# A float32 attention + two-layer MoE kernel by seven-product matrix multiplication: reordering the first four steps of the second layer

## The reference

```python
# layer 1: x = (silu(xn @ w_gate) * (xn @ w_val)) @ w_out      512 -> 1536 -> 512
# layer 2, on 2304 tokens x 512:
h = x @ w_in                                                  # 512 -> 2048
g = np.where(h >= 1, h, np.where(h <= -1, 0.0, (h + 1) ** 2 / 4.0))
out = g @ w_out                                               # 2048 -> 512
```

## Time and profile before

| | |
|---|---|
| median of 3 runs | 873.04 us (872.49 to 873.92) |
| profiled execution, its own time | 873.55 us |
| span of its instructions | 871.8 us |
| mean granted TensorE clock | 0.996 |
| PE busy | 853.6 us, 98% of the span |
| DVE / ACT busy | 659.2 us (76%) / 490.2 us (56%) |
| steps 0 to 4 of the second layer | 491.93 to 560.02 us of the span |

### The profile page before, as it was taken

One profiled execution on the slowest core, in us unless ns is written; L12 is line 12 of the kernel. 1 busy time (PEld: TensorE's weight loads), 2 busy tenths in 40 slices (PEclk: granted clock), 3 DMA queues, 4 the chain that ended last, 5 costly groups with the idle time before them and its releaser, 6 DMA issues.

```text
span 871.8 us, 17848 instructions
## 1 busy us (share of the span) xinstructions
PE 853.6 (98%) x7332; PEld 831.7 (95%) x7332; DVE 659.2 (76%) x883; ACT 490.2 (56%) x736; POOL 162.7 (19%) x107
## 2 busy tenths in 40 slices
PE   8999999999999999999999998999999999999998
PEld 5888999999999999999999997899999889999998
DVE  4698966477954976987867986766667988988884
ACT  4566654445654665644434677777778944433331
POOL 1235263345764563000000000000000000000000
PEclk9999999999999999999999999999999999999999
DMA  9993232333336335355141013242436664444442
GB/s 251 253 266 88 77 103 90 92 101 104 103 103 205 110 103 199 110 163 163 31 134 49 2 56 102 111 157 109 158 141 220 199 203 145 122 123 140 126 122 72
DMA packets 109008, 113.46 MB, mean 130 GB/s; under 512 B 6784, under 2 KB 85696, under 8 KB 108928
## 3 DMA queue, kind: packets, MB, share of 16 engines
q1 hardware_dynamic: 108928, 112.33, 41.2%
HBM read 74.55 MB, written 37.75 MB: 129 GB/s over the span
## 4 chain that ended last, share of the span: by engine, by line
PE 87%; DVE 4%; ACT 3%; DMA 2%; issue 2%; SPq 1%; DVEq 0%; ACTq 0%
PE pair L794 17%; PE pair L796 16%; PE pair L795 16%; PE pair L988 5%; PE pair L990 5%; PE pair L989 5%; PE pair L884 5%; PE pair L886 5%; PE pair L885 5%; PE pair L738 2%; PE pair L749 2%; PE pair L686 2%; PE pair L960 1%; PE pair L959 1%; PE pair L712 1%
## 5 line engine op out<-in xcount | busy, mean ns | idle before, releaser
L794 PE MATMUL pair<-xc,wc 128*128 128x288 f32 x672 | 199.5, 297 | 0.2
L795 PE MATMUL pair<-xc,wc 128*128 128x288 f32 x672 | 198.2, 295 | 0.0
L796 PE MATMUL pair<-xc,wc 128*128 128x288 f32 x672 | 197.6, 294 | 0.0
L1130 ACT ACTIVATE cp<-pair 128x576 f32<-128x576 f32 x160 | 103.5, 647 | 158.8 <-PE pair L796 151.4
L2026 POOL TENSOR_TENSOR wc<-wt,wc 128x512 fp32r<-128x512 f32 x78 | 123.2, 1603 | 117.3 <-ACT wc L1057 85.9
L794 PE MATMUL pair<-xc,wr 128*128 128x288 f32 x448 | 134.1, 299 | 8.4 <-ACT cp L1130 8.4
L795 PE MATMUL pair<-xc,wr 128*128 128x288 f32 x448 | 133.6, 298 | 0.0
L796 PE MATMUL pair<-xc,wr 128*128 128x288 f32 x448 | 133.2, 297 | 0.0
L794 PEld LDWEIGHTS pair<-xc,wc 128*128 128x128 f32 x672 | 125.9, 187 | 1.1 <-issue 0.9
L796 PEld LDWEIGHTS pair<-xc,wc 128*128 128x128 f32 x672 | 126.6, 188 | 0.0
L795 PEld LDWEIGHTS pair<-xc,wc 128*128 128x128 f32 x672 | 126.2, 188 | 0.0
(11 more groups left out here) (154 smaller groups left out, 1689.3 us busy)
## 6 DMA issues: line engine op xcount, KB each, us to landing
b_scratch<-cb SPq DMA_DIRECT2D x32, 576.0 KB, 2.9
a_scratch<-cb SPq DMA_DIRECT2D x24, 576.0 KB, 2.9
y<-a_scratch SPq DMA_DIRECT2D x16, 864.0 KB, 5.9
wt<-wB SPq DMA_DIRECT2D x72, 128.0 KB, 2.9
bt<-b_scratch SPq DMA_DIRECT2D x28, 256.0 KB, 2.8
bt<-b_scratch SPq DMA_DIRECT2D x56, 128.0 KB, 3.0
a_k<-kT SPq DMA_DIRECT2D x16, 288.0 KB, 5.7
a_q<-qT SPq DMA_DIRECT2D x16, 288.0 KB, 5.0
```

The lines of the kernel that those rows point to most:

```text
L794: pe.matmul(o, wh, xh, start=FIRST[i] and j == 0, stop=False, skip_group_check=True)
L795: pe.matmul(o, wh, xl, start=False, stop=False, skip_group_check=True)
L796: mm = pe.matmul(o, wl, xh, start=False, stop=j == 1, skip_group_check=True)
L1130: act.activation(copied(g, n)[:, :, :], pair[(X, Q, X, X)[n]][:, :, 0:HALF], ACT.Copy).then_inc(s_c, 1)
```

## The change

In steps 1 to 3 the order of ACT's and DVE's instructions is another; that of step 0 and of the steps from 4 on comes out as before. On ACT, copies 2 and 3 come ahead of the parabolas and high parts that used to stand before them: in step 1 the high parts T2, B22 and parabola 2 now follow copy 2, parabola 3 stays behind copy 3; in step 2 the four high parts and parabola 2 follow copy 2 or copy 3; in step 3 the high parts T3, T4 of tile NT+3 are made between copies 1 and 2, and parabola 1 and 2 stand between copies 2 and 3 together with the first two weight parts. DVE's order follows that of ACT. The sums of unit 13 are made in two pieces, S1 and S3 at the end of step 2, S2 and S4 in step 3.

SP issues the load of unit 13 at the same place of its queue, but waits for other things: before, for all parts of tile NT+3 (the last tile), now for the low parts of tile NT+2. What used to be behind SP's wait is waited for in two places: DVE before the sum S1, ACT before the high part A11. So that the early load writes over nothing that is still read, the last four places of the ring are used in another order (`RING_END`): the raw values of A11 and A12 go to places 9 and 10, and S1 and S2 (which DVE writes later) to 7 and 8. The places of two parts of the last product's weights (`wa21_at`) move by one accordingly. No instruction is added or taken away but semaphore waits.

```diff
--- before.py
+++ after.py
@@ -39,6 +39,7 @@
 GALL = GB + GC
 UALL = 2 * UB + UC
 RING = 11
+RING_END = (9, 7, 10, 8)
 KH = FB // 2
 NBLK = NTOK // P
 
@@ -109,7 +110,8 @@
 
 def slot_of(un, i):
 
-    return (7 * (un - 2 * UB) + i) % RING
+    n = (7 * (un - 2 * UB) + i) % RING
+    return n if n < 7 else RING_END[n - 7]
 
 
 def last_quarter(T):
@@ -193,7 +195,7 @@
 
 
         wq_at = (z_xc, z_xc + XC + 512, z_xc2, z_copy2 + 2 * 15360 + 512)
-        wa21_at = (z_w + 8 * 4096, z_w + 9 * 4096, z_raw + 512, z_cl)
+        wa21_at = (z_w + 9 * 4096, z_w + 10 * 4096, z_raw + 512, z_cl)
         wqt = [place(f"wqt{r}", [7, 2, 2, WIDE], wq_at[r]) for r in range(NGRP)]
         wa21t = [place(f"wa21t{r}", [2, 2, WIDE], wa21_at[r]) for r in range(NGRP)]
         apart = [(wa21_at[r] - wq_at[r]) // 1024 for r in range(NGRP)]
@@ -591,15 +593,13 @@
                 n = g - GB
                 if n % NT == 2 and n < GC - 2:
                     un = unit_of(g) + 1
+                    sp.wait_ge(s_wl, 7 * un)
                     if n == 2:
 
-                        sp.wait_ge(s_xh, 7 * 2 * NT)
-                        sp.wait_ge(s_xlp, 3 * 2 * NT)
-                        sp.wait_ge(s_T, 4 * 2 * NT)
+                        sp.wait_ge(s_xlp, 3 * (2 * NT - 1))
                         sp.wait_ge(s_xld, 4 * (2 * NT - 1))
                     else:
                         sp.wait_ge(s_p, 7 * (g - 2))
-                    sp.wait_ge(s_wl, 7 * un)
                     load_unit(un)
                 if n == GC - 2:
                     load_b(0)
@@ -1309,11 +1309,9 @@
                 copy(g, 0)
                 if n == 0:
                     tile_hi(NT + 1, T1)
-                if n == 2:
-                    tile_hi(NT + 3, B11)
                 if n:
                     parabola(g - 1, 0)
-                if n > 2 and n != 4:
+                if n > 4:
                     parabola(g - 1, 1)
                 copy(g, 1)
 
@@ -1322,46 +1320,58 @@
                         tile_hi(NT + 1, i)
                 if n in (1, 2):
                     parabola(g - 1, 1)
+                if n == 2:
+                    tile_hi(NT + 3, B11)
+                if n == 3:
+                    tile_hi(NT + 3, T3)
+                    tile_hi(NT + 3, T4)
+                if n == 4:
+
+                    parabola(g - 1, 1)
+                elif n > 4:
+                    parabola(g - 1, 2)
+                copy(g, 2)
+                if n == 0:
+                    tile_hi(NT + 2, B11)
                 if n == 1:
                     tile_hi(NT + 2, T2)
                     tile_hi(NT + 2, B22)
                 if n == 2:
                     tile_hi(NT + 3, T1)
                     tile_hi(NT + 3, B21)
-                if n == 4:
-
+                if n == 3:
                     parabola(g - 1, 1)
-                elif n:
-                    parabola(g - 1, 2)
-                if n == 2:
-                    tile_hi(NT + 3, T2)
-                    tile_hi(NT + 3, B22)
-                copy(g, 2)
-                if n == 0:
-                    tile_hi(NT + 2, B11)
-                if n == 1:
-                    tile_hi(NT + 2, T3)
-                    tile_hi(NT + 2, T4)
-                if n == 3:
+                    act.wait_ge(s_xlp, 3 * 2 * NT)
+                    act.wait_ge(s_T, 4 * 2 * NT)
                     unit_hi(un + 1, A11)
                     unit_hi(un + 1, S1)
+                if n in (1, 2, 3):
+                    parabola(g - 1, 2)
                 if n == 4:
                     parabola(g - 1, 2)
                 if n == GC - 3:
                     plain_w_hi(0, (0,))
                 if n == GC - 1:
                     plain_w_hi(1, (0,))
-                if n:
+                if n > 3:
                     parabola(g - 1, 3)
                 copy(g, 3)
                 if n == 0:
                     tile_hi(NT + 2, T1)
                     tile_hi(NT + 2, B21)
+                if n == 1:
+                    parabola(g - 1, 3)
+                    tile_hi(NT + 2, T3)
+                    tile_hi(NT + 2, T4)
                 if n == 2:
-                    tile_hi(NT + 3, T3)
-                    tile_hi(NT + 3, T4)
+                    tile_hi(NT + 3, T2)
+                    tile_hi(NT + 3, B22)
+                    parabola(g - 1, 3)
                 if n == 3:
-                    for i in (A12, S2, S4, S3, A22):
+                    unit_hi(un + 1, A12)
+                    unit_hi(un + 1, S2)
+                    parabola(g - 1, 3)
+                    for i in (S4, S3, A22):
                         unit_hi(un + 1, i)
                 if n in (6, 10):
                     for i in (A11, S1, A12, S2):
@@ -1493,6 +1503,10 @@
             def unit_sum(un, s):
                 if s == S1:
                     dve.wait_ge(d_w[un % 2], 128 * (un // 2 + 1))
+                    if un == 2 * UB + 1:
+                        dve.wait_ge(s_xh, 7 * (2 * NT - 1) + B22 + 1)
+                        dve.wait_ge(s_xlp, 3 * 2 * NT)
+                        dve.wait_ge(s_T, 4 * 2 * NT)
                     dve.tensor_tensor(w_raw(un, S1), w_a21(un), w_raw(un, A22), ALU.add).then_inc(s_S, 1)
                 if s == S3:
                     if un >= 2 * UB:
@@ -1889,27 +1903,25 @@
             for g in range(GB, GALL):
                 un, n = unit_of(g), g - GB
                 if n == 2:
-                    tile_sums(NT + 3)
-                    token_lo(NT + 3, B11)
-                    token_lo(NT + 3, T1)
-                if n == 1 or n > 2:
+                    tile_sum(NT + 3, T1)
+                    tile_sum(NT + 3, T2)
+                if n:
                     joined(g - 1, 0)
-                if n == 3:
-                    unit_sums(un + 1)
                 c11(g)
                 if n == 0:
                     for i in range(B21, T4 + 1):
                         token_lo(NT + 1, i)
+                if n == 3:
+                    unit_sum(un + 1, S2)
+                    unit_sum(un + 1, S4)
+                else:
+                    if n:
+                        joined(g - 1, 1)
+                    if n > 3:
+                        joined(g - 1, 2)
                 if n == 2:
-                    joined(g - 1, 0)
-                    token_lo(NT + 3, B21)
-                if n:
-                    joined(g - 1, 1)
-                if n in (1, 2):
-                    token_lo(NT + 1 + n, T2)
-                    token_lo(NT + 1 + n, B22)
-                if n:
-                    joined(g - 1, 2)
+                    tile_sum(NT + 3, T3)
+                    tile_sum(NT + 3, T4)
                 if n in (GC - 3, GC - 1):
                     wq_sum((n - (GC - 3)) // 2, S1)
                     wq_sum((n - (GC - 3)) // 2, S3)
@@ -1917,27 +1929,53 @@
                 if n == 0:
                     tile_sums(NT + 2)
                 if n == 1:
-                    token_lo(NT + 2, T3)
-                    token_lo(NT + 2, T4)
+                    token_lo(NT + 2, T2)
+                    token_lo(NT + 2, B22)
+                if n == 2:
+                    token_lo(NT + 3, B11)
+                    token_lo(NT + 3, T1)
+                    token_lo(NT + 3, B21)
+                if n in (1, 2):
+                    joined(g - 1, 2)
+                if n == 3:
+                    unit_lo(un + 1, A11)
+                    unit_lo(un + 1, S1)
+                    joined(g - 1, 1)
                 if n in (6, 10):
                     unit_sums(un + 1)
-                if n in (3, 7, 11):
-                    for i in {3: (A11, S1)}.get(n, (A12, S2)):
+                if n in (7, 11):
+                    for i in (A12, S2):
                         unit_lo(un + 1, i)
-                if n:
+                if n > 3:
                     joined(g - 1, 3)
                 c22_c21(g)
                 if n == 0:
                     for i in (B11, T1, B21):
                         token_lo(NT + 2, i)
+                if n == 1:
+                    joined(g - 1, 3)
+                    token_lo(NT + 2, T3)
+                    token_lo(NT + 2, T4)
                 if n == 2:
+                    token_lo(NT + 3, T2)
+                    token_lo(NT + 3, B22)
+                    joined(g - 1, 3)
+                    unit_sum(un + 1, S1)
+                    unit_sum(un + 1, S3)
                     token_lo(NT + 3, T3)
                     token_lo(NT + 3, T4)
+                if n == 3:
+                    unit_lo(un + 1, A12)
+                    unit_lo(un + 1, S2)
+                    joined(g - 1, 2)
+                    joined(g - 1, 3)
+                    for i in (S4, S3, A22):
+                        unit_lo(un + 1, i)
                 if n in (6, 10):
                     unit_lo(un + 1, A11)
                     unit_lo(un + 1, S1)
-                if n in (3, 7, 11):
-                    for i in {3: (A12, S2, S4, S3, A22)}.get(n, (S4, S3, A22)):
+                if n in (7, 11):
```

(1 more changed line is left out.)

## The result

The changed kernel takes 861.59 us in the median (860.49 to 864.14, 4 runs) against 872.95 of the kernel before in the same measurement: ratio 0.9873, 95% interval 0.9849 to 0.9896. Forecast were 862.0 us and a range of 860.8 to 864.6. Two later measurements of the same kernel gave 861.73 (ratio 0.985, 0.9819 to 0.9881) and 861.87 (0.9866, 0.9841 to 0.9891).

What follows compares the result with a forecast made beforehand. PE, busy 98%, bounds the kernel; its waits, restarts and half clock in steps 0 to 4 lose 12.09 us. With 1.04 still lost, 11.05 is won: 873.04 - 11.05 = 862.0 us, range 860.8 to 864.6.

Steps and rivals of the forecast that it cites:

- The 12.09 us that could be won: Steps 0 to 4 of the second layer: time lost to PE's three waits, restarts and half clock, the most to gain.
- Step 1 and 2: Copy 2 of step 1 at 509.95, copy 3 at 513.02; no PE wait in either step.
- The load: Unit 13's weights: issued about 517.5, landed 524.8, needed by DVE's S1 about 529.2, so 4.4 us of cover.
- the thin place of the prediction: `c11` of step 3 at 532.55, after step 1's second store lands at about 532.3: 0.2 us of cover.
- the bound for a landing behind the load: Stores land 2.9 us after issue, 4.4 at worst, which would hold DVE 1.3 us.
- Steps 3 and 4: PE waits 0.53 us for copy 3 of step 3, about 0.3 more in step 4, plus restarts of 0.08.
- The clock: Half clock after two waits of the kernel before cost some 1.5 us each, 3.0 together; afterwards 1.00 throughout.
- the first two waits: Kernel before: PE waits 1.97 us before step 1, product 5 and 4.27 before step 2, product 5; both go.
- The rival that small waits lower the clock: Up to five small waits within one step lower the granted clock; one stretch costs 1.5 us: 863.5 us; chance 0.07.
- A full wait at step 3 or 4: Rival: ACT's queue between copies 2 and 3 of step 3 slips, costing 2.15 us or more: 864 to 865.7; chance 0.11.
- That the changed kernel's gain is owed later: Rival that the change does nothing: step 4 or 5 gives the gain back, 872 to 874 us; chance 0.05.
- The slower rival: Step 1's store, now behind the load, lands late and `c11` of step 3 holds DVE and PE: 875 us; chance 0.03.

Runs made afterwards that it cites:

- the last order tried: Changed kernel with ACT's and DVE's order of steps 3 and 4 also carried on, work that may follow a copy put behind it: 861.08 us, ratio 0.9861.
- the order alone: Kernel before with the new ACT and DVE order in steps 1 and 2 only, step 3 and the load as before: 869.55 us, ratio 0.9956.
- the renumbered kernel: Kernel before with only the last four ring places, and the two places of the last product's weights, in another order: 873.37 us, ratio 0.9987.
- the load alone: Kernel before with only the earlier load of unit 13, its ring places and waits; ACT and DVE in the old order: 870.11 us, ratio 0.9952.

## Why the prediction was right

*The 12.09 us that could be won.* Right: 191.29 - 12.09 = 179.20, and the last order tried came to 179.44.

*Step 1 and 2.* Right in each mark: copy 2 of step 1 started 18.01 after the layer's start (forecast 509.95 - 491.93 = 18.02), copy 3 at 21.08 (21.09). No wait in either step.

*The load.* Issued 25.6 after the layer's start (forecast 25.6). Its cover held, S1 had no wait, but it was thinner than forecast: the load's last DMA, issued at 521.72, landed at 524.93, which is 34.4 after the layer's start where 524.8 - 491.93 = 32.9 was forecast, so the cover was 2.9 us and not 4.4. `c11` of step 3 was the thin place of the prediction; it did not wait, and the second store of step 1 landed 0.33 us before it (forecast 0.2). `c11` of step 4 waited 0.17 for a store, which the prediction had not named. What the order alone showed is that the bound for a landing behind the load was too low: 5.8 us, not 4.4. In the changed kernel the second store of step 1 is issued at 528.0, 5.6 us after the first and 6.2 after the load's last DMA, it landed after 2.9 us, and nothing waited for it.

*Steps 3 and 4.* 0.54 and 0.26 of waits and two restarts against 0.53 and 0.3; the whole loss 0.97 against 1.04. The reason given (4.36 us of work between copies 2 and 3, the backlog at copy 2 of step 4) was tested by moving that work behind the copies: the loss fell to 0.15.

*The clock.* Here the sum was right for the profiled execution and right by luck for the others. It took 3.0 us for two stretches at the lower level after the first two waits. The profile of the renumbered kernel had one in these steps, with nearly the same waits. One such stretch of 3.4 us takes 3.4 x 0.5 / 870 = 0.002 off an execution's mean clock; 31 runs of the kernel before had means between 0.990 and 0.998, 0.9946 on average, so an estimated (1 - 0.9946) / 0.002 = 2.7 stretches each, while those of the changed kernel lay between 0.998 and 1.000. Not all of the 2.7 need follow the three waits: the two stretches at 77 to 84 and 80 to 87 us in other profiles, where nothing was changed, count for two each. So the clock's part of the gain is an estimated 2.7 x 1.5 = 4 us or less, less what a later wait gives back, and it differs from run to run. The rival that small waits lower the clock is out for the profiled executions: 0.38, 1.87 and 2.67 us did not. By the Trainium skill's price for a stretch (TensorE: Matmul & The Clock Gate, HAM oscillation: its length times (1 - 1.2/2.4)) the gain would have been an estimated 11.4; measured in the layer's steps are 11.07, nearer to the rows' 11.05. The forecast did not hang on this price, though the prediction says so: the 12.09 us are a difference of starts, whatever the clock's share in them, and with 1.7 for a stretch the terms would have come to 12.5, more than was there. Matmuls at the lower level stood 0.24 us apart, not twice 0.133, which is why 3.4 us of it cost 1.5.

*The rivals.* A full wait at step 3 or 4 did not stay. That the changed kernel's gain is owed later is out by the last stage, which starts 11.07 us sooner after the second layer's start and takes no longer than before. The slower rival's mechanism exists (1.5 us in one experiment), but it cost nothing in this kernel.

What stays open: what decides whether the clock falls after a wait of 2 us, and why it fell at about 80 us in two profiles. Waits of the same length at other times were not tried.

## What to carry to other kernels

Where one engine frees another's accumulators, work out for each copy the earliest start and the latest harmless one; in a queue kept in order, everything that may wait belongs behind the copy whose window is narrow, and durations from the profile placed the copies here to a tenth of a microsecond. Where two causes make waits in one stretch, taking away either alone can give much less than its share of the whole: with the order alone PE only came sooner to the missing weights, with the load alone the copies were late as before; the two gave 1.7 and 2.2 us less waiting apart, and 8.0 together. And a load that is moved in a DMA queue moves all stores behind it: look at who waits for these.

## What was not expected of the hardware

The granted clock fell after 1.97 us of waiting in one execution and stayed at 1.00 after 1.87, 1.95, 2.15, 2.67 and 2.95 in others; it fell at each wait of 4.27 us or longer. After waits of 1.97 and 4.27 the lower level held for 3.4 us; with one of 6.3 it held for 6.8 and with one of 7.1 for 10.2, and in these two it began before PE went on. A store of 576 KB that normally lands 2.9 us after its issue took 4.0 right behind the eight DMAs of a 1 MB load in the changed kernel, and 5.8 where it was the second of two such stores that followed them at once (4.4 in the kernel before).
